# Exponents of the first two tiles from a row with ones, and the splitting of the first weight chunks regrouped, in an mLSTM and two-layer gated MLP kernel

## What is computed

```python
def _attn_ref(q, k, v, i_gate, f_gate, o_gate):
    for t in range(S):
        m_new = np.maximum(f_gate[:, :, t] + m, i_gate[:, :, t])
        f_stab = np.exp(f_gate[:, :, t] + m - m_new)
        i_stab = np.exp(i_gate[:, :, t] - m_new)
        m = m_new
        C = f_stab * C + i_stab * outer(vt, kt)
        n = f_stab * n + i_stab * kt
        y[:, :, t] = sigmoid(o_gate_t) * (C @ qt) / max(abs(n . qt), 1)

x = rows(y)                                        # (1536, 320)
x = (sigmoid(x @ w_gate) * (x @ w_val)) @ w_out    # layer 0, 320 -> 1536 -> 320
xn = x / rms(x) * rms_g
y = (silu(xn @ w_gate2) * (xn @ w_val2)) @ w_out2  # layer 1
```

## Time and profile before

| | us |
|---|---|
| median of 3 runs | 452.12 (452.08 to 452.18) |
| the profiled execution | 452.08 |
| its span | 450.3 |
| PE busy | 444.9 |
| DVE busy | 211.3 |
| ACT busy | 186.8 |
| POOL busy | 97.0 |

### The profile page before, as it was taken

The page is one execution under the profiler, slowest core; times in us unless marked ns, Lnnn a source line. Parts: engine busy times, 40 slices in busy tenths (PEclk is TensorE's granted clock), DMA queues, the critical chain, the costliest instruction groups (busy, mean ns, idle before and its releaser), DMA issues.

```text
span 450.3 us, 10548 instructions
## 1 busy us (share of the span) xinstructions
PE 444.9 (99%) x4489; PEld 404.2 (90%) x4489; DVE 211.3 (47%) x465; ACT 186.8 (41%) x355; POOL 97.0 (22%) x141
## 2 busy tenths in 40 slices
PE   8999999999999999999999999999999999999997
PEld 3799999999999999988889988889988899888897
DVE  8746746854476356424332217561055630256510
ACT  8976367554654463215544144231032320133310
POOL 2999711012101200013656172000000000000000
PEclk9999999999999999999999999999999999999999
DMA  7684600210221012100443110000000000000000
GB/s 253 208 264 136 206 3 1 77 62 17 75 75 58 22 45 90 70 1 2 121 132 102 44 45 1 1 0 31 31 2 0 1 16 29 16 1 2 0 31 29
DMA packets 10127, 25.91 MB, mean 58 GB/s; under 512 B 1376, under 2 KB 4480, under 8 KB 10080
## 3 DMA queue, kind: packets, MB, share of 16 engines
q1 hardware_dynamic: 9760, 25.15, 17.2%
q10 hardware_dynamic: 320, 0.08, 0.1%
HBM read 23.18 MB, written 1.97 MB: 56 GB/s over the span
## 4 chain that ended last, share of the span: by engine, by line
PE 95%; DVE 2%; POOL 2%; issue 0%; ACT 0%; POOLq 0%; DVEq 0%
PE bank L1097 36%; PE bank L1113 10%; PE bank L1115 9%; PE bank L1114 9%; PE bank L1046 8%; PE bank L1047 8%; PE bank L1049 5%; PE bank L965 2%; PE bank L996 2%; PE bank L899 2%; PE bank L984 1%; POOL wgv_lo L435 1%; PE bank L939 1%; PE bank L1005 1%; DVE first L832 1%; POOL wgv_hi L440 0%
## 5 line engine op out<-in xcount | busy, mean ns | idle before, releaser
L1097 PE MATMUL bank<-x_hi,wgv_hi 64*128 64x512 f32 x576 | 105.8, 388 | 0.0
L620 ACT ACTIVATE sg<-bank 128x256 f32<-128x256 f32 (+1 forms) x96 | 47.1, 492 | 131.0 <-PE bank L1097 82.3
L1097 PE MATMUL bank<-x_lo,wgv_hi 64*128 64x512 f32 x480 | 93.9, 386 | 0.0
L853 DVE TENSOR_TENSOR bank<-sg,bank 128x256 f32<-128x256 f32 (+1 forms) x96 | 53.8, 561 | 67.2 <-ACT sg L620 65.6
L1046 PE MATMUL bank<-x_hi,wgv_hi 128*128 128x256 f32 x288 | 80.5, 290 | 0.4 <-POOL wgv_hi L440 0.4
L1047 PE MATMUL bank<-x_lo,wgv_hi 128*128 128x256 f32 x288 | 78.3, 282 | 0.0
L1113 PE MATMUL bank<-wo_hi,h_hi 128*128 128x320 f32 x240 | 75.4, 314 | 0.0
L1097 PE MATMUL bank<-x_hi,wgv_lo 64*128 64x512 f32 x384 | 75.1, 386 | 0.0
L1115 PE MATMUL bank<-wo_hi,h_lo 128*128 128x320 f32 x240 | 74.1, 309 | 0.0
L1114 PE MATMUL bank<-wo_lo,h_hi 128*128 128x320 f32 x240 | 74.1, 309 | 0.0
L1097 PEld LDWEIGHTS bank<-x_hi,wgv_hi 64*128 64x128 f32 x576 | 54.4, 184 | 11.5 <-issue 0.7
(11 more groups left out here) (125 smaller groups left out, 546.8 us busy)
## 6 DMA issues: line engine op xcount, KB each, us to landing
step<-in_vok SPq DMA_DIRECT2D x12, 324.0 KB, 3.2
step<-in_qk_t SPq DMA_DIRECT2D x24, 160.0 KB
step<-in_w_gv SPq DMA_DIRECT2D x6, 576.0 KB, 3.9
raw_p<-in_w_gv SPq DMA_DIRECT2D x5, 576.0 KB, 3.9
raw_x<-in_w_gv SPq DMA_DIRECT2D x5, 576.0 KB, 5.0
step<-in_vok SPq DMA_DIRECT2D x10, 160.0 KB, 4.2
raw_x<-in_w_o SPq DMA_DIRECT2D x3, 480.0 KB, 3.5
raw_p<-in_w_o SPq DMA_DIRECT2D x3, 480.0 KB, 3.5
```

The source lines that it names most:

```text
L620: act.activation(sg_view(n), g_view(n), ACT.Sigmoid).then_inc(sg_done, 1)
L853: dve.tensor_tensor(v_view(n), sg_view(n), v_view(n), ALU.mult).then_inc(hf_done, 1)
L1097: mm = pe.matmul(ps(n), w, x, start=own and (s, p) == (0, 0), stop=last and not own)
```

## The change

PE: 11 idle matmuls instead of 21; then the masks of both tiles, then for each head of a tile one matmul of 128 columns, `d_rhs` (a row pattern of ones) times `l_row`, into the same banks, then the 512-column matmul with a smaller left side. The scores of tiles 0 and 1 go into banks of their own and no longer wait for the exponentials; K comes after T; `hidden(0, 0)` comes before D 2 and D 3, starts when both x_hi are there, takes its x_lo products last in the gate half, and the hidden tiles wait for each chunk by itself.

DVE: `d_rhs0` and its two products are gone. Part 0's rows are reordered, of part 1's rows only the scans stand ahead of the weighing of tile 0; the rest stands behind x_lo of tile 1, and after the copies K comes `l_end` and `split_third(2)`, the whole split of chunk 2.

POOL: fills the lower half of `d_lhs` (64x1280) and half of `d_rhs`' lower half (64x1024) after its patterns; splits chunk 0 before D 0, chunk 1 after D 1 in thirds of 128 columns, with a wait for `lhs_done` behind the first third, then chunk 3; chunk 2 is no longer its work. ACT: fills less, takes chunk 0's high part before D 0 and one copy of tile 1's sums between D 0 and D 1, chunks 2 and 3 after T 1.

SP: `raw0` 0 is loaded before q and k, kn before `raw0` 2, and the waits on `split0` count in thirds for chunk 1 (`split_by_pool`); the slot of chunk 2 is free with `split2`. Chunk 4 waits for all thirds of chunk 1. Ring banks are renumbered.

```diff
-        d_rhs0 = first[0][:, 0:R * P].rearrange("p (r t) -> p r t", t=P)
-        d_lhs0 = first[1][:, 0:P]
+        d_lhs0 = first[1][0:2 * Q, 0:P]
...
+        def split_by_pool(c, i=FC - 1):
+            return 1 if c == 0 else 2 + i if c == 1 else c + 2
...
# SP
             def load_raw0(c):
-                if c >= len(raw0):
-                    sp.wait_ge(split0, c - len(raw0) + 1)
+                if c - len(raw0) == 2:
+                    sp.wait_ge(split2, 1)
+                elif c >= len(raw0):
+                    sp.wait_ge(split0, split_by_pool(c - len(raw0)))
...
+            load_raw0(0)
             load_qk(0)
             load_qk(1)
             load_vo(0)
-            load_raw0(0)
...
+            load_vo(2)
+            load_kn(2)
             load_raw0(4)
-            load_vo(2)
             load_raw0(5)
...
# POOL
-                               pattern=[[HALF, 2], [-1, P]], channel_multiplier=1).then_inc(hide_done, 1)
+                                    pattern=[[HALF, 2], [-1, P]], channel_multiplier=1))
+            pool.tensor_copy(d_lhs[HALF:P, :, :, :], hide[HALF:P, :, :].unsqueeze(1).to_broadcast([HALF, NJ - 1, 2, P])
+                             ).then_inc(hide_done, 1)
+            pool.wait_ge(hide_done, 1)
+            pool.tensor_copy(d_rhs[HALF:P, H:R, :].rearrange("p r (u t) -> p r u t", u=2),
+                             ident[HALF:P, HALF:P].unsqueeze(1).unsqueeze(1).to_broadcast([HALF, H, 2, HALF])
+                             ).then_inc(fill1_done, 1)
...
-            pool.wait_ge(high_done, 2)
+            pool.wait_ge(high1_done, 1)
...
+            split(0, 0)
             piece(("D", 0))
             piece(("D", 1))
-            for c in range(4):
-                split(0, c)
+            split_gv(0, 1, slice(0, P))
+            pool.wait_ge(lhs_done, 1)
+            for i in range(1, FC):
+                split_gv(0, 1, slice(i * P, (i + 1) * P))
+            split(0, 3)
             piece(("D", 2))
...
# ACT
+            high(0, 0)
             piece(("D", 0))
+            act.wait_ge(sums_done, 1)
+            act.activation(l_row[0:R, P:2 * P], l_r[:, P:2 * P], ACT.Copy).then_inc(high1_done, 1)
             piece(("D", 1))
-            high(0, 0)
...
             high(0, 1)
-            high(0, 2)
-            act.wait_ge(hide_done, 1)
-            act.activation(d_lhs[HALF:P, :, :, :], hide[HALF:P, :, :].unsqueeze(1).to_broadcast([HALF, NJ - 1, 2, P]),
-                           ACT.Copy).then_inc(fill_done, 1)
             piece(("T", 0))
             piece(("T", 1))
+            high(0, 2)
+            high(0, 3)
...
# DVE
+            def split_third(c):
+                r = raw_of(0, c)
+                dve.wait_ge(whi0, c + 1)
+                dve.tensor_tensor(wgv_lo[:, c, 0, :], r[:, 0, :], wgv_hi[:, c, 0, :].bitcast(F32), ALU.subtract)
+                link(dve.tensor_tensor(wgv_lo[:, c, 1, :], r[:, 1, :], wgv_hi[:, c, 1, :].bitcast(F32), ALU.subtract))
+                dve.tensor_tensor(wgv_hi[HALF:P, c, 2, :], r[HALF:P, 2, :], wgv_hi[HALF:P, c, 2, :].bitcast(F32),
+                                  ALU.subtract).then_inc(split2, 1)
...
-            for b in range(B):
-                dve.tensor_tensor(d_rhs0[0:2 * Q, H * b:H * b + H, :],
-                                  l_row[:, 0:P].bitcast(F32).unsqueeze(1).to_broadcast([2 * Q, H, P]),
-                                  sel[0:2 * Q, b, :].unsqueeze(2).to_broadcast([2 * Q, H, P]), ALU.mult).then_inc(drhs_done, 1)
-            for sub in range(5):
+            for sub in range(2):
                 rows(1, sub)
...
             for n in range(B):
                 piece(("T", n))
+            rows(1, 2)
+            rows(1, 3)
             for n in range(B):
                 piece(("K", n))
+            dve.wait_ge(consts, 1)
+            rows(1, 4)
+            split_third(2)
...
# PE
-            idle(bank[6], 20)
-            idle(bank[3], 1)
-            for kind in "DS":
-                for n in range(B):
-                    piece((kind, n))
-            idle(bank[7], 4)
+            idle(bank[6], 11)
+            pe.wait_ge(consts, 2)
+            for n in range(B):
+                for i in range(2):
+                    pe.matmul(bank[exp_base(n) + i][:, :], ident_b[:, :], causal[:, :].unsqueeze(1).to_broadcast([P, 4, P]),
+                              start=True, stop=False)
+            pe.wait_ge(rows_done, 1)
+            for n in range(B):
+                pe.wait_ge(fill_done, n + 1)
+                for h in range(H):
+                    pe.matmul(bank[exp_base(n) + h // 4][:, h % 4 * P:(h % 4 + 1) * P], d_rhs[0:HALF, H * n + h, :],
+                              l_row[:, 0:P], start=False, stop=False)
+            pe.wait_ge(lhs0_done, 1)
+            for n in range(B):
+                for i in range(2):
+                    r0 = H * n + 4 * i
+                    pe.matmul(bank[exp_base(n) + i][:, :], d_lhs0, d_rhs[0:HALF, r0:r0 + 4, :].rearrange("p q t -> p (q t)"),
+                              start=False, stop=True).then_inc(d_done, 1)
...
             piece(("T", 1))
+            for n in range(B):
+                piece(("K", n))
+            hidden(0, 0)
             piece(("D", 2))
             piece(("D", 3))
-            hidden(0, 0)
             piece(("R", 1))
```

More of the change, by code:

```diff
@@ L266, in mlstm_moe_kernel @@
         init_done = sem("init_done")
-        selc_done = sem("selc_done")
         hide_done = sem("hide_done")
         fill_done = sem("fill_done")
+        fill1_done = sem("fill1_done")
+        sums_done = sem("sums_done")
+        high1_done = sem("high1_done")
+        lhs0_done = sem("lhs0_done")
         high_done = sem("high_done")
@@ L313, in mlstm_moe_kernel @@
         split0 = sem("split0")
+        split2 = sem("split2")
         whi1 = sem("whi1")
@@ L716, in rows @@
-                    link(dve.tensor_tensor(i_r[:, cs], i_r[:, cs], m_r[:, cs], ALU.subtract))
+                        last = dve.tensor_tensor_scan(l_r[:, js], ones[:, :], f_r[:, js], 0.0, ALU.mult, ALU.add)
+                    if part == 0:
+                        link(last)
+                        dve.tensor_copy(l_row[0:R, ls], l_r[:, cs]).then_inc(high_done, 1)
+                        dve.tensor_tensor(i_r[:, cs], i_r[:, cs], m_r[:, cs], ALU.subtract)
+                        dve.wait_ge(high_done, 1)
+                        dve.tensor_tensor(l_row[Q:Q + R, ls], l_r[:, cs], l_row[0:R, ls].bitcast(F32),
+                                          ALU.subtract).then_inc(rows_done, 1)
+                    elif part == 1:
+                        last.then_inc(sums_done, 1)
+                        dve.wait_ge(sums_done, 1)
@@ L717, in rows @@
                 elif sub == 2:
+                    if part:
+                        link(dve.tensor_tensor(i_r[:, cs], i_r[:, cs], m_r[:, cs], ALU.subtract))
+                    else:
+                        dve.wait_ge(rows_done, 1)
                     link(dve.tensor_tensor(i_r[:, cs], i_r[:, cs], l_r[:, cs], ALU.subtract))
                     if part == 0:
-                        dve.tensor_copy(d_lhs0[2 * Q:2 * Q + R, :], i_r[:, cs])
-                    else:
-                        dve.tensor_copy(d_lhs[0:R, j0 - 1:j1 - 1, :, :], halves(i_r[:, cs]))
@@ L723, in rows @@
-                    if j0 >= LR:
-                        dve.wait_ge(flat_in, 32 * (j1 - 1 - LR))
-                    dve.tensor_copy(l_row[0:R, ls], l_r[:, cs]).then_inc(high_done, 1)
+                        link(dve.tensor_copy(d_lhs0[0:R, :], i_r[:, cs]))
+                        dve.tensor_tensor(d_lhs0[Q:Q + R, :], i_r[:, cs], d_lhs0[0:R, :].bitcast(F32),
+                                          ALU.subtract).then_inc(lhs0_done, 1)
+                        return
+                    high = dve.tensor_copy(d_lhs[0:R, j0 - 1:j1 - 1, :, :], halves(i_r[:, cs]))
@@ L1044, in hidden @@
                     wc = 2 * c + m
-                    for s in range(3):
-                        pe.matmul(ps, wgv_hi[:, wc, s, cs], x_hi[:, xs, s, :], start=(s == 0), stop=False)
-                        mm = pe.matmul(ps, wgv_hi[:, wc, s, cs], x_lo[:, xs, s, :], start=False, stop=(s == 2))
-                        if s < 2:
-                            pe.matmul(ps, wgv_lo[:, wc, s, cs], x_hi[:, xs, s, :], start=False, stop=False)
+                    if k == 0 and wc == 2 and i == 0:
+                        pe.wait_ge(split2, 1)
+                    elif k == 0 and (i == 0 or wc == 1):
+                        pe.wait_ge(split0, split_by_pool(wc, i if wc == 1 else FC - 1))
+                    passes = [(s, p) for s in range(3) for p in ((0, 1, 2) if s < 2 else (0, 1))]
+                    if n == 0:
+                        passes = [sp for sp in passes if sp[1] != 1] + [sp for sp in passes if sp[1] == 1]
+                    for s, p in passes:
+                        if n == 0 and m == 0 and p == 1:
+                            pe.wait_ge(x_done, B)
```

(4 more changed lines are left out.)

163 lines of the change are left out of this document (85 added, 78 removed).

## The result

| | before | after |
|---|---|---|
| median, us (16 executions each) | 452.10 (452.07 to 452.18) | 453.13 (452.70 to 453.56) |
| the profiled execution | 452.08 | 452.80 |
| its span | 450.3 | 451.0 |

The ratio of after to before is 1.0022, with a 95% interval of 1.0014 to 1.0030. The changed kernel is 1.03 us slower by the medians, where the forecast said 0.4. The profiled execution is one of the quick ones of its kernel: 0.72 us above before's. The profile has to explain the 0.72. The other 0.3 is spread between executions, of which the new kernel has 0.86 us and the old 0.11.

A forecast was written before the change was run, and what follows sets the result against it. TensorE, busy 99% of the span, was taken as the bound. Its 2.0 us lead is lost: chunk 4 starts 1.0 us later, turns cost 0.45, and PE resumes at 55.1 instead of 54.70: 452.08 + 0.4 = 452.5, range 450.8 to 453.9.

The forecast's parts named there:

- same: Whole kernel: a result within 0.9 us of no change, given 0.51; faster was given 0.22, slower 0.27.
- Rival 4: Chunk 4's landing takes 5.0, giving 453.3, or products take 0.23 each, giving 454.4; chance 0.15.
- Bound and slack: Before the tenth hidden tile: PE waits for POOL's chunk 11, which has 1.0 us of slack; PE resumes at 55.1.
- Ports at the start: Prologue: POOL's copies (1.2 and 1.0 us) and VectorE's rows block each other; first exponential near 8.75 against 8.63.
- rival 1: Ports matter less: exponents 0.4 earlier, chunks 1 and 11 not stretched; 451.1, or 450.6 with a 3.7 landing; chance 0.17.
- rival 3: Prologue: POOL's copies hold VectorE longer, 4.4 instead of 2.2 us, giving 454.7; chance 0.11.
- rival 2: Chunk 4's data is not what POOL waits for, all of PE's 2.0 us lead stays, 450.1; chance 0.05.
- Cost nothing as long as `rows_done` is no earlier: Start of PE: the 11 idle and four mask matmuls end near 6.0 and cost nothing under that condition.
- PE's lead: At `hidden(0, 1)`: PE arrives at 20.5 instead of 22.5, 2.0 us ahead.
- Chunk 1: POOL's split, slowed 0.6 us by VectorE's chunk 2 work, is whole at 22.7; chunk 4 loads after, landing in 4.2.
- Turns inside chunk 11: With PE ahead, VectorE's scan falls in the middle of POOL's chunk 11 and the two take turns: 0.45 us.
- VectorE took chunk 2 and that brings nothing: Before chunk 4: POOL is spared 3.1 us without gain, as it waits for chunk 4's data.

The follow-up runs named there:

- experiment 7: Kernel before with one POOL memset (about 0.75 us) added ahead of chunk 4: median 452.17, ratio 1.0002.
- experiment 8: Kernel before with three POOL memsets (about 2.25 us) added ahead of chunk 4: median 453.35, ratio 1.0030.
- experiment 4: Changed kernel with POOL's two copies into d_lhs and d_rhs moved behind a wait for sums_done: median 452.89, ratio 1.0027.
- experiment 1: Changed kernel without POOL's wait for lhs_done ahead of chunk 1's last two thirds: median 453.05, ratio 1.0025.
- experiment 2: Changed kernel with tile 2's exponentials ahead of chunk 3's high half on ACT: median 453.38, ratio 1.0038.
- experiment 5: Changed kernel with chunk 3 loaded before q and k of tiles 2 and 3: median 452.82, ratio 1.0026.
- experiment 6: Changed kernel with chunk 3 loaded before q and k of tiles 2 and 3, and no POOL wait for lhs_done: median 451.65, ratio 1.0001.
- experiment 3: Changed kernel without POOL's wait for lhs_done and with tile 2's exponentials ahead of chunk 3's high half: median 452.77, ratio 1.0022.
- experiment 11: Changed kernel, chunk 3 loaded before q and k, lhs_done wait behind chunk 1's second third, more idle matmuls before the two transposes: median 451.48, ratio 0.9993.
- experiment 12: Changed kernel with chunk 2 split by POOL, between chunks 1 and 3, instead of by VectorE: median 453.61, ratio 1.0038.
- experiment 9: Changed kernel, chunk 3 loaded before q and k of tiles 2 and 3, lhs_done wait behind chunk 1's second third: median 451.67, ratio 0.9994.

## Why the prediction was right, and where it was not

The outcome lies in the range (450.8 to 453.9), and it is slower, as forecast. Where PE stands still and what it waits for there was named; of what makes chunk 4 late only one half was, the load, and not ACT. The size is 1.03 and not 0.4, just over the 0.9 us that the text took as the border of "same", so it fell in the part that was given 0.27 and not in the one given 0.51. The sum for the profiled execution was 0.4 against 0.72, and that it came so near is in part luck: two terms cancelled. Rival 4's 453.3 is nearer to the median, by chance: neither a landing of 5.0 nor products of 0.23 occurred.

- *Bound and slack: right.* PE stands still before the tenth hidden tile, released by POOL's L474, at 55.37 (forecast 55.1). The slack of 1.0 measured as 0.9 to 1.0 in experiments 7 and 8.
- *Ports at the start: right in cause and size.* Copies 1.32 and 1.04 (1.2 and 1.0), VectorE's rows 1.25 and 1.06, exponentials at 8.85 (8.75). The rule that was quoted from the Trainium skill ("SBUF — State Buffer", Who interferes with whom) held. Rivals 1 and 3 fall by these rows, rival 2 by chunk 4, which starts later than before (28.78), and rival 4 with a landing of 3.76 us and products of 0.115. In experiment 4, without the blocking, the exponentials came no earlier, so of rival 1's first 0.4 us between 0 and 0.35 was to be had: the idle and mask matmuls end near 6.2 in after and at 6.5 there, where "near 6.0" was forecast. "Cost nothing as long as `rows_done` is no earlier" was true of after by 0.35 us, and it left out that the idle matmuls take 4.05 us in one execution, 4.50 in another, 4.87 in a third.
- *PE's lead: a term left out, and mis-sized.* Forecast 2.0 us at `hidden(0, 1)`, measured 1.04. About 0.4 of the difference is a slip in the sum: to the start at 17.2 it added the hidden tile (2.1) and D 2 and D 3 (1.2), and not R 1, which also stands ahead of `hidden(0, 1)` (21.05 to 21.43 in after). A start 2.8 us earlier less 1.2 is a lead of 1.6. The rest is a later start: weighing began at 10.70 and not 10.2, x ended at 18.31 and not 17.8, and `hidden(0, 0)` began at 17.86 and not 17.2. The half microsecond comes from ahead of the weighing: the products start 0.2 later, and the four 512-column matmuls take 1.07 us (8.38 to 9.45) and not 0.92. From there to the last x_lo the chain takes the forecast 7.6 us.
- *Chunk 1: mis-sized.* Whole at 23.7 and not 22.7: `lhs_done` 0.5 later, and turns with VectorE's three instructions on chunk 2. The first of the two remaining thirds took 2.52 us, the second, undisturbed, 1.41: 1.1 us lost against 0.6 in the sum, inside its bounds of 0.4 and 1.2. The landing was 3.76 and not 4.2 and gave 0.4 back; chunk 4 at 28.78, forecast 28.2.
- *ACT: missed, the step that failed most.* The prediction moved chunk 3's high half ahead of tile 2's exponentials without asking when its data would land behind the loads of q and k. It cost ACT 1.46 us, PE two waits of 0.35, and the lead. Experiments 1, 2, 5 and 6 show that this and the late load each suffice to hold chunk 4: one alone gives 0.1, 0.3 or less than nothing, both give 1.5 (experiment 6; 0.4 by the median of experiment 3).
- *Turns inside chunk 11: 0.45 foreseen, zero in after,* because PE had lost its lead and the scan (54.61) fell behind most of chunk 11. Where the scan falls into the middle of chunk 11 either side pays: POOL in experiments 11 (0.44) and 12 (0.33, chunk 11 lasts 3.13), the scan itself in 6 and 9 (1.39 and 1.40). So the sum had 0.6 us too little before chunk 4, 0.1 too little from there to chunk 11 and 0.45 too much in chunk 11; the first and the last are the two terms that cancelled.
- *"VectorE took chunk 2 and that brings nothing": wrong.* Experiment 12 puts it at 0.5 us by the medians. The sentence compared POOL's end of chunk 3 with chunk 4's data in the new kernel, where VectorE had already done the work, instead of adding the 3.1 us back.
- *The spread: not in the sum.* The last 0.3 us between the profiled execution and the median come with the 0.86 us of spread, against 0.11 before. One source is visible at the start: in ten profiles of after and its variants the 11 idle matmuls took 4.05 to 4.87 us, and where they took over 4.5 the products came late (6.54 in after, 6.92 in 12, 7.14 in 3), while in before 0.48 us of waiting for VectorE stood behind the 21, and 0.39 and 0.42 in two later waits, to take such shifts up. In experiment 7 the 21 took 7.43 us instead of 6.22 and the scores came 0.34 later, yet `hidden(0, 0)` started at 20.09 instead of 20.02. The two slowest profiles against their own medians (5 and 12, 0.6 and 0.7 above) had 4.87 and 4.86, the quickest (9, 0.7 below) 4.19; but 3 had 4.87 and lay 0.2 below, and 2 had 4.69 and lay 0.5 below. So it is a part at most, and no experiment isolated it. What puts single executions at 0.989 stays open too: no profile fell into one.

The best of these kernels are 6, 9 and 11, with medians 0.4 to 0.6 us below before and best executions 0.5, 1.1 and 1.0 us below; since the intervals of their ratios include 1, a gain over before is not shown.

## What to carry to other kernels

When a prologue becomes shorter, list for the first transfer behind it every release that stands there, the load's and that of each engine's queue, and when the data of everything moved ahead will land. Two late releases side by side make every single repair look useless (here +0.3, -0.1 and -0.3 us alone, all within the spread, and -1.5 in the better of the two pairs), so test pairs before a cause is dropped. A lead on the busiest engine is worth nothing beyond the slack of the slowest supply chain, and that slack can be measured by adding work of known length in front of that chain.

## What the runs showed of the hardware

The same 576 KB load (chunk 3) landed after 3.6 to 3.9 us in before (issued 3.9 us after the last load of q and k) and in experiments 5, 6, 9 and 11 (issued ahead of them), and after 5.6 to 6.9 us in after and in experiments 1 to 4 and 12, where those of two tiles were issued 1.6 to 1.8 us ahead of it. Of a VectorE and a GpSimd instruction that both read two operands from SBUF either can be the one that waits: the scan in experiment 9 (1.40 instead of 0.73), chunk 11 in experiment 11 (3.24 instead of 2.80), with scans that start only 0.05 us apart and chunk 11 0.15. TensorE, after standing still for 2.70 us, ran the next matmuls at the lower of its levels (1.2 GHz; granted clock 0.53 from 7.90 to 11.30 us, 0.88 us a pair instead of 0.46), while in after the products that follow 0.35 us of standing still are 0.115 us apart. The 11 idle matmuls at the start of after and its variants took between 4.05 and 4.87 us in ten profiles.
